# Strided and local attention in blocks of 64 keys instead of tiles of up to 128, ahead of two MoE stages

## The chip, the cores and the metric

The kernel runs as one program on one core of a Trainium2 chip. The metric is the device time of one execution in microseconds (us). The core has TensorE (PE; its weight loads are listed as PEld), VectorE (DVE), ScalarE (ACT) and GpSimd (POOL), which run side by side and are ordered by semaphores alone, and a sync queue (SP) that issues most DMA transfers.

## The reference

Three stages follow each other, all in fp32. The change is in the first.

```python
B, H, S, D = 4, 8, 576, 64
scores = (q @ k.transpose(0, 1, 3, 2)) / sqrt(D)
rel = pos[:, None] - pos[None, :]
mask_local = (rel >= 0) & (rel < 32)                        # heads 0 to 3
mask_strided = (rel >= 0) & (pos[None] % 32 == pos[:, None] % 32)   # heads 4 to 7
attn = softmax(where(mask, scores, -1e9))                   # sum + 1e-9
x = (attn @ v), heads side by side: (2304, 512)
# MoE: 8 experts, top 1, 512 -> 1024 -> 512, tokens with x @ w_skip <= 0 pass through
# then x @ w_in (512 x 2048), a piecewise activation, @ w_out (2048 x 512)
```

A query of a local head sees at most 32 keys. A query of a strided head sees the positions up to its own in its class modulo 32, at most 18. The host lays the strided heads out by class, so that the 18 positions of a class are neighbours and the mask is a block diagonal of 18 by 18 triangles.

## The kernel before, in words

Attention takes a tile of queries against a tile of keys for the four heads of one kind. A local tile is 96 queries against the 128 keys from 32 before them, 6 tiles a batch. A strided tile holds 6 or 5 classes (`CLASSES`), that is 108 or 90 queries against the same 108 or 90 keys, 6 a batch. Two neighbouring tiles are the work of one step (`TWINS`), so a batch has `TB` = 6 steps and the kernel 24.

For each step TensorE does four things. `scores` writes the mask (0 or -8e9) into the score banks by 4 bf16 matmuls against an identity and adds 8 matmuls q·k over 64 partitions; the two halves `hh` of the partitions hold two heads. `turn` transposes the 8 weight blocks, 4 a tile, into `probT_b`. `values` does 8 matmuls of 64 weight columns (the head's dimension) against the transposed weights into `out_b[i % 2]`. Round s of `steps` does `turn(s - 3)`, `scores(s)`, `values(s - 3)` in this order (`LAG` = 3). The first five rounds and the last are written out, the others are a loop with six rounds in its body.

Around it, for step n: VectorE takes the negative row maxima of the 8 blocks (line 604), scales them (606), adds 1e-9 to the sums (611), inverts them (613) and copies the transposed weights to `probT` (620). ScalarE does 8 exponentials with bias and accumulated sum (489) and places the output in `XT` (497); for strided tiles the destination is scattered, one element in 32. GpSimd multiplies the weights by the inverse sums, once a tile (407). The scores of step n wait for the exponentials of step n - 2 (two pairs of banks), `values(n)` for the placing of step n - 2 (two output banks).

The sync queue loads q and k of the local heads, v of the local heads, then the same of the strided heads, each into a single buffer; a buffer of the next batch is requested when the last step that reads it has been scored or multiplied. The routing (logits from line 868 on), the experts (927, 937) and the last stage (970, 983) follow in order on TensorE. The first routing matmul waits for the placing copy of the last step.

The change touches the constants at the top, the buffers of attention, the sync queue's loads, the loops of all five engines over the steps, and the masks of `host_constants`.

## Time and profile before

| what | value |
|---|---|
| time, median of 3 runs | 706.28 us (704.29 to 706.91) |
| the profiled execution, its time | 704.93 us |
| its span, first to last instruction | 703.2 us |
| mean granted clock of TensorE | 0.963 of full speed |
| busy share: TensorE, VectorE, ScalarE, GpSimd | 93%, 47%, 33%, 21% |
| bytes moved by DMA | 73.95 MB |

The span is 1.7 us shorter than the time of the same execution. A busy share is a mean over the whole span; attention is about its first 93 us, and there the shares differ much from the rest. In the profile "x16" counts instructions; an fp32 matmul of the code appears as two of them, a transpose or a bf16 matmul as one. The clock column gives the share of 2.4 GHz that TensorE was granted; 0.5 is 1.2 GHz.

### The profile page before, as it was taken

Reading aid. Unit: us, or ns where it says so; the run is one execution under the profiler, and the core shown is the slowest. Engines: PE = TensorE matmul, PEld = TensorE weight load, DVE = VectorE, ACT = ScalarE, POOL = GpSimd, SP = SyncE. Lnnn points to the kernel's source line nnn. Section 1 sums busy time; section 2 is a strip of 40 time slices with the busy share of each in tenths; the row PEclk is TensorE's granted clock in tenths of the full one; section 3 lists DMA queues with packets and bytes.
Section 4 is the critical chain, followed back from the end, with each engine's and each line's share of the span. In section 5 each row is a group of like instructions: output and inputs, shape, how many; then the busy total and the mean of one; then the engine's idle time right before and its main releaser. Section 6 shows DMA issues by size and latency. Waiting matters only on the chain.

```text
span 703.2 us, 11023 instructions
## 1 busy us (share of the span) xinstructions
PE 657.1 (93%) x4149; PEld 567.4 (81%) x4149; DVE 330.2 (47%) x614; ACT 229.0 (33%) x693; POOL 149.3 (21%) x163
## 2 busy tenths in 40 slices
PE   7999892299999999989999999999999999999995
PEld 4877762299999999968888888888888888888994
DVE  3877733032111112387445644456445564455653
ACT  4999932032111111122223322233222332222331
POOL 1655506302221222785000200002000020000201
PEclk8999977599999999999999999999999999999998
DMA  8565166693777776222000100001000010000100
GB/s 259 180 214 207 40 255 261 225 394 126 265 263 248 262 264 225 88 94 60 1 1 0 61 1 0 1 0 60 0 0 0 0 60 0 0 0 1 61 1 30
DMA packets 37854, 73.95 MB, mean 105 GB/s; under 512 B 2739, under 2 KB 16224, under 8 KB 37808
## 3 DMA queue, kind: packets, MB, share of 16 engines
q1 hardware_dynamic: 34936, 63.92, 26.3%
q0 software_dynamic: 2880, 9.52, 3.5%
q8 instruction: 24, 0.39, 0.2%
q14 instruction: 14, 0.11, 0.1%
HBM read 63.49 MB, written 9.94 MB: 104 GB/s over the span
## 4 chain that ended last, share of the span: by engine, by line
PE 82%; ACT 6%; DMA 4%; POOL 3%; issue 2%; DVE 2%; SPq 0%; DVEq 0%
PE pair L970 28%; PE pair L983 15%; PE bank L983 12%; PE pair L927 10%; PE bank L937 9%; ACT prob L489 5%; DMA WE<-w 2%; POOL x_sorted L418 2%; PE bank L841 1%; PE bank L827 1%; PE bank L911 1%; PE pair L814 1%; PE bank L868 1%; DMA k_loc<-kT 1%; ACT XT L497 1%
## 5 line engine op out<-in xcount | busy, mean ns | idle before, releaser
L970 PE MATMUL pair<-yh,WIH 128*128 128x512 f32 (+1 forms) x320 | 116.5, 371 | 0.2 <-ACT yh L548 0.2
L970 PE MATMUL pair<-yh,WIL 128*128 128x512 f32 (+1 forms) x320 | 116.3, 370 | 0.0
L572 ACT ACTIVATE cl<-cl,half 128x512 f32<-128x512 f32 (+1 forms) x80 | 54.5, 681 | 187.2 <-DVE cl L768 187.2
L477 POOL DMA_INDIRECT out<-XT,tok x18 | 18.8, 1045 | 351.6 <-DVE XT L756 347.7
L776 DVE TENSOR_TENSOR gl<-gr,gh 128x512 fp32r<-128x512 f32 (+1 forms) x80 | 56.3, 703 | 73.1 <-ACT gh L581 71.9
L768 DVE TENSOR_SCALAR cl<-pair 128x512 f32<-128x512 f32 (+1 forms) x80 | 50.9, 637 | 71.0 <-PE pair L970 70.8
L970 PE MATMUL pair<-yl,WIH 128*128 128x512 f32 (+1 forms) x320 | 79.9, 370 | 2.1 <-DVE yl L747 2.1
L927 PE MATMUL pair<-xw,WE 128*128 128x168 f32 x512 | 75.7, 310 | 0.3 <-DMA WE<-w 0.3
L927 PEld LDWEIGHTS pair<-xw,WE 128*128 128x128 f32 x512 | 74.5, 193 | 0.7 <-DMA WE<-w 0.6
L581 ACT CAST gh<-gr 128x512 fp32r<-128x512 f32 (+1 forms) x80 | 46.3, 578 | 85.7 <-PE bank L983 58.3
L937 PE MATMUL bank<-hid,WE 128*128 128x168 f32 x512 | 74.1, 306 | 0.0
L937 PEld LDWEIGHTS bank<-hid,WE 128*128 128x128 f32 x512 | 73.3, 190 | 0.0
L970 PEld LDWEIGHTS pair<-yh,WIH 128*128 128x128 f32 x320 | 60.8, 190 | 11.3 <-ACT yh L548 0.6
L970 PEld LDWEIGHTS pair<-yh,WIL 128*128 128x128 f32 x320 | 60.7, 190 | 10.6
L489 ACT ACTIVATE prob<-pair,sm 96x128 f32<-96x128 f32 (+2 forms) x192 | 65.7, 419 | 10.5 <-DVE sm L606 9.4
L970 PEld LDWEIGHTS pair<-yl,WIH 128*128 128x128 f32 x320 | 57.0, 189 | 13.0 <-DVE yl L747 3.1
L774 DVE TENSOR_TENSOR gr<-gr,cl 128x512 f32<-128x512 f32 (+1 forms) x80 | 52.6, 657 | 22.6 <-ACT cl L572 22.6
L983 PE MATMUL pair<-WOH,gh 128*128 128x512 f32 x160 | 62.5, 391 | 0.0
L983 PE MATMUL pair<-WOL,gh 128*128 128x512 f32 x160 | 62.4, 390 | 0.0
L983 PE MATMUL pair<-WOH,gl 128*128 128x512 f32 x160 | 62.3, 389 | 0.0
L728 DVE TENSOR_TENSOR ytmp<-bank,gb 128x168 f32<-128x168 f32 x32 | 10.6, 333 | 105.6 <-PE bank L937 105.6
L529 ACT ACTIVATE hid<-pair 128x168 f32<-128x168 f32 x64 | 19.9, 310 | 109.7 <-PE pair L927 109.7
(124 smaller groups left out, 933.7 us busy)
## 6 DMA issues: line engine op xcount, KB each, us to landing
WE<-w SPq DMA_DIRECT2D x16, 2048.0 KB, 9.1
xrow<-x_sorted SPq DMA_DIRECT2D x6, 781.5 KB, 10.5
raw_in<-win SPq DMA_DIRECT2D x16, 256.0 KB, 9.2
raw_out<-wout SPq DMA_DIRECT2D x16, 256.0 KB, 2.5
v_loc<-vl SPq DMA_DIRECT2D x4, 768.0 KB, 5.1
q_str<-qT SPq DMA_DIRECT2D x4, 576.0 KB, 5.8
k_str<-kT SPq DMA_DIRECT2D x4, 576.0 KB, 6.8
q_loc<-qT SPq DMA_DIRECT2D x3, 576.0 KB, 4.6
```

Of the source, the lines that this page charges most:

```text
L477: pool.indirect_dma_start(out, bass.IndirectOffsetOnAxis(tok[:, GT * g + t:GT * g + t + 1], 0), rows_of(g, t), None).then_inc(out_done if ...
L489: last = act.activation(prob[0:q, i % 3, e * kk:(e + 1) * kk], score_b[i % 2][0:q, e // 4, e % 4 * kk:(e % 4 + 1) * kk], ACT.Exp, bias=sm[ ...
L529: act.activation(hid[:, par, f, :], hid_b[f % 2][:, 0:WIN], ACT.Relu).then_inc(h_done, 1)
L572: act.activation(cl[:, 0:n], cl[:, 0:n], ACT.Square, bias=half[:, :], scale=0.5).then_inc(squared, 1)
L581: act.copy(gh[:, f % 2, 0:n], gr[:, 0:n]).then_inc(g_high, 1)
L768: dve.tensor_scalar(cl[:, 0:n], h2_b[f % 2][:, 0:n], -1.0, 1.0, ALU.max, ALU.min).then_inc(clamped, 1)
L774: dve.tensor_tensor(gr[:, 0:n], gr[:, 0:n], cl[:, 0:n], ALU.add).then_inc(g_ready, 1)
L776: dve.tensor_tensor(gl[:, f % 2, 0:n], gr[:, 0:n], gh[:, f % 2, 0:n].bitcast(F32), ALU.subtract).then_inc(g_low, 1)
L927: last = pe.matmul(hid_b[f % 2][:, 0:WIN], WE1[:, par, c, P * f:P * (f + 1)], xw[:, buf, c, :], start=(c == 0), stop=(c == DC - 1))
L937: last = pe.matmul(y_b[c][:, 0:WIN], WE2[:, par, f, P * c:P * (c + 1)], hid[:, par, f, :], start=(f == 0), stop=(f == FEC - 1))
L970: last = pe.matmul(h2_b[f % 2][:, 0:tokens], w[:, c, P * f:P * (f + 1)], x[:, c, 0:tokens], start=(k == 0), stop=(k == 3 * DC - 1))
L983: last = pe.matmul(fin_b[t][:, :], x[:, f % 2, P * t:P * (t + 1)], w[:, f, :], start=(f == 0 and k == 0), stop=(f == FFC - 1 and k == 2))
```

## The change

Attention is cut differently. Keys come in blocks of 64 (`KEYS`). Local queries come in blocks of 32 (`BLOCK`), each against the 64 keys that end with them; strided queries in strips of 3 classes, 54 queries (`STRIP`), against 64 keys of which 54 are their own. A step now holds for each of 4 heads two halves `j` of 64 key columns, and in each half the rows of 2 strips, of 4 local blocks, or of a mix (the rest step: one strip, one local block, one single class). So the score tile is always 128 rows by 8 x 64 columns. A batch has 5 steps: two of strips, one rest, two of blocks; the kernel has 20.

- TensorE: 4 mask matmuls of 128 columns a step; 16 score matmuls in a step of strips, 24 in the rest step, 32 in a step of blocks, each of 64 moving columns and 54, 18 or 32 weight columns; 4 transposes of 128 by 128; as many value matmuls as score matmuls, each over 64 partitions with 64 weight columns and 54, 32 or 18 moving columns. The values of step n come in round n + 4, one round after its transposes.
- ScalarE: one exponential over 512 elements from SBUF; the copy of the transposed weights; the placing, in one to three copies.
- VectorE: row maxima of the scores, a subtraction of the maxima from the scores into `prob`, a sum of the exponentials, the add of 1e-9 and the inverse.
- GpSimd: one multiplication a step.
- Score banks: two pairs, used in the order 0, 1, 0, 0, 1 over the five steps; a pair is free once it has been subtracted. The output has one pair of banks instead of two single ones. `prob` has five slots, `probT` three, `probT_b` one bank.
- Loads: strided q and k first, whole inputs per batch in single buffers, v of the local heads (1 MB instead of 0.77) later than before, v of the rest step apart. Constants and the MoE gate's weights are requested during the second batch.
- The loops over steps of ScalarE, VectorE, GpSimd and of the sync queue are written out; TensorE's is a loop with five rounds in its body.

```diff
+BLOCK, KEYS = 32, 64
+BLOCKS = S // BLOCK
+STRIP = 3 * PHASE
+PAIR = 2 * STRIP
...
+SCORES_IN = [0, 1, 0, 0, 1]
+TB = len(TILES_OF)
+STEPS = B * TB
...
-LAG = 3
+SLOTS = TB
+LAG, LAST = 3, 4
...
+            for b in range(1, B):
+                done = TB * (b - 1)
+                sp.wait_ge(scored, done + REST_STEP + 1)
+                load_qk_strided(b)
+                if b > 1:
+                    sp.wait_ge(pv_done, done)
+                    load_v_local(b - 1)
+                sp.wait_ge(scored, done + TB)
+                load_qk_local(b)
+                sp.wait_ge(pv_done, done + STRIPS_B + 1)
                 load_v_strided(b)
+                sp.wait_ge(pv_done, done + REST_STEP + 1)
+                load_v_rest(b)
...
+            for n in range(STEPS):
                 pool.wait_ge(inverted, n + 1)
...
+                pool.tensor_tensor(weights, weights, sm[:, n % SLOTS, 24:32].unsqueeze(2).to_broadcast([P, 8, KEYS]), ALU.mult).then_inc(normed, 1)
...
+            def exps(n):
+                act.wait_ge(lowered, n + 1)
+                act.activation(prob[:, n % SLOTS, :], prob[:, n % SLOTS, :], ACT.Exp, scale=SCALE).then_inc(probs_done, 1)
+
+            def copy_turned(n):
+                act.wait_ge(turned, n + 1)
+                behind(act, pv_done, n - 1)
+                act.copy(probT[:, TURNED_IN[n % TB], :], probT_b[:, :]).then_inc(turn_copied, 1)
...
+            for s in range(STEPS + LAST):
+                if 0 <= s - 1 < STEPS:
+                    exps(s - 1)
+                if 0 <= s - LAG < STEPS:
+                    copy_turned(s - LAG)
+                if 0 <= s - LAST:
+                    place(s - LAST)
...
+                dve.tensor_reduce(small[:, 0:8].rearrange("q (h g) -> q h g", h=2), scores, AX_X, ALU.max).then_inc(maxed, 1)
                 dve.wait_ge(maxed, n + 1)
...
+                dve.tensor_tensor(prob[:, n % SLOTS, :].rearrange("q (h g k) -> q h g k", g=4, h=2), scores,
+                                  small[:, 0:8].rearrange("q (h g) -> q h g", h=2).unsqueeze(3).to_broadcast([P, 2, 4, KEYS]), ALU.subtract).then_inc(lowered, 1)
...
+            def scores_of(i, hh):
+
+                out = score_b[SCORES_IN[i]][:, hh, :]
+                half_ = slice(KEYS * hh, KEYS * hh + KEYS)
+                for j, (mask, _) in enumerate(TILES_OF[i]):
...
+                for j, (_, parts) in enumerate(TILES_OF[i]):
+                    for p in range(2):
+                        for x in parts:
+                            queries, keys = (q_str, k_str) if x.kind == "s" else (q_loc, k_loc)
+                            col = P * p + KEYS * j
+                            yield pe.matmul(out[x.row:x.row + x.queries, col:col + KEYS], queries[half_, p, x.first:x.first + x.queries], keys[half_, p, x.keys:x.keys + KEYS],
+                                            start=False, stop=(j == 1 and p == 1), skip_group_check=True)
...
+                behind(pe, lowered, n if i == BLOCKS_A else n - 1)
+                for _, last in zip(scores_of(i, 0), scores_of(i, 1)):
+                    pass
...
+                for g in range(4):
+                    last = pe.transpose(probT_b[:, P * g:P * (g + 1)], prob[:, i, P * g:P * (g + 1)], ident)
...
+                pe.wait_ge(turn_copied, n + 1)
+                behind(pe, x_placed, n)
...
+                for p in range(2):
                     for hh in range(2):
...
+                        for pair in zip(*(parts for _, parts in TILES_OF[i])):
+                            for j, x in enumerate(pair):
+                                half_, h = slice(KEYS * j, KEYS * (j + 1)), 2 * p + hh
...
+                                last = pe.matmul(out_b[KEYS * hh:KEYS * (hh + 1), j, to:to + x.queries], vv[half_, x.index, HD * h:HD * (h + 1)],
+                                                 probT[half_, TURNED_IN[i], from_:from_ + x.queries], start=True, stop=True)
...
+                if turning:
+                    turn(*turning[:2])
+                if scoring and i != BLOCKS_A:
+                    scores(n, i, b)
+                if valuing:
+                    values(*valuing)
+                if scoring and i == BLOCKS_A:
+                    scores(n, i, b)
```

## Rows read from the trace of the kernel before

**Rows 1.** The page: its busy shares, and one line of its DMA issues.

```profile
PE 657.1 (93%) x4149; PEld 567.4 (81%) x4149; DVE 330.2 (47%) x614; ACT 229.0 (33%) x693; POOL 149.3 (21%) x163
...
k_str<-kT SPq DMA_DIRECT2D x4, 576.0 KB, 6.8
```

**Rows 2.** The chain that ended last: start us, length us, what.

```profile
49.94 1.58 ACT prob L489 x9
...
69.26 1.58 ACT prob L489 x9
...
92.08 0.77 ACT XT L497
...
169.00 9.12 PE bank L937 x64
```

**Rows 3.** Busy time of each engine by stretches of attention.

```profile
core 0: us, PE busy (x) PEld busy (x) DVE busy (x) ACT busy (x) POOL busy (x), PEclk, DMA share, GB/s
...
0.00:9.70 9.70, 6.05 (x30) 2.63 (x30) 2.17 (x6) 1.88 (x4) 1.06 (x8) 0.96 0.75 234
9.40:16.00 6.60, 6.26 (x43) 4.90 (x44) 1.85 (x5) 4.28 (x26) 1.35 (x2) 0.52 1.04 330
16.00:87.00 71.00, 67.44 (x956) 55.75 (x954) 55.94 (x135) 69.87 (x382) 40.95 (x45) 1.00 0.47 161
87.90:98.00 10.10, 8.98 (x68) 4.70 (x68) 1.31 (x4) 1.54 (x2) 0.96 (x2) 0.52 0.45 165
```

**Rows 4.** Timeline of TensorE over one step: start us, length us, instruction.

```profile
29.07 0.60 PE L806 MATMUL pair<-mask_b,ident_b 96*96 96x256 bf16 x4
...
29.60 1.12 PE L814 MATMUL pair<-k_loc,q_loc 64*96 64x128 f32 x16
...
30.65 0.84 PE L841 MATMUL bank<-probT,v_str 90*64 90x90 f32 x16
...
31.42 0.82 PE L827 MATMUL bank<-con,prob 90*90 90x90 f32 x8
...
32.19 0.42 PE L806 MATMUL pair<-mask_b,ident_b 96*96 96x256 bf16 x2
```

**Rows 5.** Timeline of four TensorE groups without their first pair or record.

```profile
39.55 0.73 PE L814 MATMUL pair<-k_str,q_str 64*90 64x90 f32 x14
...
36.31 0.83 PE L814 MATMUL pair<-k_str,q_str 64*108 64x108 f32 x14
...
30.78 0.71 PE L841 MATMUL bank<-probT,v_str 90*64 90x90 f32 x14
...
31.54 0.71 PE L827 MATMUL bank<-con,prob 90*90 90x90 f32 x7
```

**Rows 6.** Timeline: a group's first two weight loads, then its first four.

```profile
36.13 0.17 PEld L814 LDWEIGHTS pair<-k_str,q_str 64*108 64x108 f32 x2
...
36.13 0.27 PEld L814 LDWEIGHTS pair<-k_str,q_str 64*108 64x108 f32 x4
...
40.20 0.14 PEld L841 LDWEIGHTS bank<-probT,v_loc 128*64 128x64 f32 x2
...
40.20 0.20 PEld L841 LDWEIGHTS bank<-probT,v_loc 128*64 128x64 f32 x4
```

**Rows 7.** Groups by line and shape: busy us, mean ns of one, idle before.

```profile
L407 POOL TENSOR_TENSOR prob<-prob,sm 96x512 f32<-96x512 f32 x24 | 24.5, 1039 | 27.8 <-DVE sm L613 27.8
...
L604 DVE TENSOR_REDUCE sm<-pair 96x8 f32<-96x1024 f32 x12 | 14.7, 1221 | 13.1 <-PE pair L814 13.1
...
L868 PE MATMUL bank<-XT,wgs 128*32 128x512 f32 x32 | 5.9, 906 | 0.9 <-ACT XT L497 0.9
...
L497 ACT COPY XT<-bank 128x360 f32 x6 | 5.0, 840 | 0.0
...
L613 DVE RECIPROCAL sm<-sm 96x8 f32<-96x8 f32 x12 | 2.4, 199 | 0.4
...
L572 ACT ACTIVATE cl<-cl,half 128x512 f32<-128x512 f32 x64 | 46.3, 724 | 166.2 <-DVE cl L768 166.2
L774 DVE TENSOR_TENSOR gr<-gr,cl 128x512 f32<-128x512 f32 x64 | 45.7, 715 | 17.2 <-ACT cl L572 17.2
```

More of the change, by code:

```diff
@@ L1 @@
+import itertools
+from collections import namedtuple
 from contextlib import ExitStack
@@ L222, in program @@
         block = ctx.enter_context(nc.Block())
-        STEPS = B * TB
-        FIRST = LAG + 2
-        LOOPS = (STEPS - FIRST) // TB
-        def steps(eng, step, lag):
-            for s in range(FIRST):
-                step(s, s, 0)
-            with eng.Fori(0, LOOPS) as b:
-                for i in range(TB):
-                    step(FIRST + i, TB * b + (FIRST + i), b)
-            for s in range(FIRST + LOOPS * TB, STEPS + lag):
-                step(s, s, 0)
         def rows_of(g, t):
@@ L615, in copy_turned @@
-            def copy_turned(n, i):
-                behind(dve, pv_done, n)
-                for j in range(2):
-                    q, kk, _, _, _, _ = TWINS[i][j]
-                    dve.wait_ge(turned, 2 * n + j + 1)
-                    dve.tensor_copy(probT[0:kk, j, 0:4 * q], probT_b[j][0:kk, 0:4 * q]).then_inc(turn_copied, 1)
-            def step(k, s, b):
-                for lag, work in ((LAG, copy_turned), (0, maxima), (1, inverses)):
-                    m = s - lag
-                    if isinstance(m, int) and not 0 <= m < STEPS:
-                        continue
-                    work(m, (k - lag) % TB)
@@ L629, in _ @@
-            steps(dve, step, LAG)
+                dve.tensor_scalar(small[:, 16:24], small[:, 8:16], 1e-9, None, ALU.add).then_inc(guarded, 1)
+                dve.wait_ge(guarded, n + 1)
+                dve.reciprocal(small[:, 24:32], small[:, 16:24]).then_inc(inverted, 1)
+            for s in range(STEPS + 1):
+                if s < STEPS:
+                    maxima(s)
+                if s >= 1:
+                    inverses(s - 1)
             done = [0]
@@ L818, in turn @@
-            def turn(n, i, b):
-                for j in range(2):
-                    q, kk, _, _, _, _ = TWINS[i][j]
-                    pe.wait_ge(normed, 2 * n + j + 1)
-                    behind(pe, turn_copied, 2 * n + j - 1)
-                    for hh in range(2):
-                        for p in range(2):
-                            e, h = 4 * hh + 2 * j + p, 2 * hh + p
-                            last = pe.transpose(probT_b[j][0:kk, h * q:(h + 1) * q], prob[0:q, i % 3, e * kk:(e + 1) * kk], ident[0:q, 0:q])
-                    last.then_inc(turned, 1)
@@ L845, in step @@
-            def step(k, s, b):
-                for lag, work in ((LAG, turn), (0, scores), (LAG, values)):
-                    m = s - lag
-                    if isinstance(m, int) and not 0 <= m < STEPS:
-                        continue
-                    work(m, (k - lag) % TB, b + (k - lag) // TB)
-            steps(pe, step, LAG)
+            def scores_of(i, hh):
+                out = score_b[SCORES_IN[i]][:, hh, :]
+                half_ = slice(KEYS * hh, KEYS * hh + KEYS)
+                for j, (mask, _) in enumerate(TILES_OF[i]):
+                    pe.matmul(out.rearrange("q (p j k) -> q p j k", p=2, j=2)[:, :, j], ident_b[:, :], mask_b[:, mask, :].unsqueeze(1).to_broadcast([P, 2, KEYS]),
+                              start=(j == 0), stop=False, skip_group_check=True)
+                    yield
+                for j, (_, parts) in enumerate(TILES_OF[i]):
[5 more added lines that the diff above has]
+                                            start=False, stop=(j == 1 and p == 1), skip_group_check=True)
@@ new lines, in round_of, with step @@
+            def round_of(scoring, turning, valuing):
+                n, i, b = scoring
+                if turning:
[6 more added lines that the diff above has]
+                    scores(n, i, b)
+            def step(s):
+                return (s, s % TB, s // TB) if 0 <= s < STEPS else None
+            for s in range(FIRST):
+                round_of(step(s), step(s - LAG), step(s - LAST))
@@ L855, in _ @@
+            with pe.Fori(0, LOOPS) as b:
+                for k in range(FIRST, FIRST + TB):
+                    round_of(*((TB * b + k - lag, (k - lag) % TB, b + (k - lag) // TB) for lag in (0, LAG, LAST)))
+            for s in range(STEPS, STEPS + LAST):
+                if step(s - LAG):
+                    turn(*step(s - LAG)[:2])
+                values(*step(s - LAST))
             pe.wait_ge(wg_in, 16)
```

289 lines of the change are left out of this document (148 added, 141 removed).

## The prediction

> **What bounds the kernel now.** I read the busy shares first [rows 1]: TensorE is busy 93% of the span, but as an average over stages with different limits. The chain of waits [rows 2] then places the change: attention ends with the placing copy at 92.08 + 0.77 = 92.85 us, and the routing matmuls start right behind it. All after that (703.2 − 92.85 = 610.3 us) is untouched and hangs on that copy, so the question is only when attention ends. Between the same point of two batches lie 69.26 − 49.94 = 19.32 us for 6 steps, 3.22 us a step, and the chain stands there on ScalarE's exponentials. The table by stretches [rows 3] shows that two engines share this limit: from 16 to 87 us ScalarE is busy 69.9 and TensorE 67.4 of 71 us, VectorE 55.9, GpSimd 41.0. A gain on ScalarE alone would buy almost nothing: TensorE's own work in a step, from one mask matmul to the next, is 32.19 − 29.07 = 3.12 us [rows 4]. So the sum must be made on TensorE.
>
> **How TensorE's work is priced.** An fp32 matmul of the code leaves two records (8 matmuls are x16 [rows 4]). Alone, a record of 168 columns takes 9.12/64 = 0.1425 us [rows 2], two clock cycles a column at 2.4 GHz. Matmuls on different halves of the array run side by side: scores and values go in pairs of records, and a pair of 90 columns takes (0.71 − 0.24)/6 = 0.078 us [rows 5], the time of one transpose record of 90 columns (last row, 0.078). With 90 weight columns the pair takes (0.73 − 0.24)/6 = 0.082, with 108 (0.83 − 0.26)/6 = 0.095. The weight loads say what limits small ones [rows 6]: the second pair of loads comes 0.10 us behind the first for 108 weight columns, 0.06 for 64. That is about 0.9 ns a column for a pair, twice one load at 2.4 GHz, beside a matmul or not.
>
> **The change, part by part.**
>
> *ScalarE.* Eight exponentials with their accumulator reads, which with one placing copy fill today's step, become one over 512 elements: 0.72 us by the 512-element activation [rows 7]. It takes over from VectorE the copy of the transposed weights (512 elements too, 0.72 at most) and keeps the placing; 360 scattered elements take 0.84 [rows 7], so two copies of 216 about 1.0. Worst step 2.5 us.
>
> *VectorE.* The maximum falls from 1.22 us (1,024 elements) to about 0.69 by its slope of one element per 1.04 ns [rows 7]; added are a subtraction of 512 (0.72), a sum of 512 (0.69), and the small add and the reciprocal remain (0.2 each [rows 7]). With handovers 2.5 us a step. GpSimd's two multiplications of 1.04 [rows 7] become one. None of these three reaches TensorE's new time below, and that is the work that hides them; they bound the step at 2.5 us from below.
>
> *TensorE.* Steps fall from 24 to 20, but a batch has 120 score and 120 value matmuls where it had 48 and 48: 480 records, 96 a step on average (64 in steps of strips, 96 in the rest step, 128 in blocks), against 32. Fixed parts of a step:
> - 4 mask matmuls of 128 columns: half of 0.108, 0.22 us.
> - 4 transposes of 128 columns: 0.078 × 128/90 = 0.11 each, 0.44 (before 0.62).
> - Four changes between groups. Four groups cost 3.12 us, of which 4 × 0.108 + 8 × 0.109 (their columns at 2.4 GHz) + 8 × 0.078 + 8 × 0.078 = 2.55 is pace; 0.57 is change. I take 0.53.
>
> Together 1.19. The value records carry 64 weight columns and only 32 or 54 moving ones, so the load decides: 0.06 a pair, 0.029 a record (they go through two halves at a time). It is bounded below by the moving columns (0.0145 for 32) and above by today's pace, 0.039. The score records carry 32 or 54 weight columns for 64 moving ones. If no more than a pair overlaps, they cost (64 × 2/2.4 + 3)/2 = 0.028; but the code walks them over 4 tiles of the array in strips and 8 in blocks, and four tiles do overlap in this trace: 32 records of 512 columns are done in 5.9 us, mostly at 1.2 GHz, where one alone would take 0.85 [rows 3, 7]. Then loads set 0.013 to 0.025. I take 0.0145, since that row is the nearest to it, and keep 0.028.
>
> P, the step, is 1.19 + 48 × 0.029 + 48 × 0.0145 = 3.28 us. So the step is no shorter than before; the gain comes from having four fewer of them and from ends.
>
> The Trainium skill, page "TensorE: Matmul & The Clock Gate", section "Wait — 56ns, not 53.3ns?", says that matmuls never start closer than some 25 ns however few their columns. The trace shows pairs starting almost together, but none of its averages is under 39 ns, so it doesn't decide. By that figure the step would be 1.19 + 48 × 0.029 + 48 × 0.025 = 3.78 us, close to the pairs-only rival.
>
> *Values one round behind.* Values of step n now follow a round after its transposes, so the copy between them hides behind a whole round of TensorE. That this buys much is excluded by TensorE's idle time, 3.6 us in 71 for all waits together [rows 3]; and it costs nothing while ScalarE has the time. The one output pair makes a loop: values (at most 1.9), last matmul's latency 0.25, placing 0.6 to 1.0, 0.2 of handovers: 2.9 at most, under P with the turn and scores between. The scores of the first block step reuse the rest step's banks and wait for VectorE's 1.45 us; turn and values (1.9) stand ahead of them. Hidden; if that cover went, 1 us a batch.
>
> *Loads.* 4.2 MB a batch instead of 3.6, in 5P = 16.4 us: 258 GB/s. Queries and keys (1.15 MB) have 2.7 rounds, 8.9 us, between their release and need; the later of the two lands 6.8 us after issue in the median [rows 1]. Hidden. The sync queue waits between them for events of earlier rounds alone.
>
> *The ends.* Start: before, the second step began when 1.40 MB of requests had landed, at 9.7 us. Now its data is as much, but the third step needs 2.53 MB: at the 330 GB/s of that stretch [rows 3], 3.4 us later, 13.1. At half clock (0.52 there) its scores end near 15.5, VectorE lowers them 1.5 us later, and the fourth step's scores end near 18.3. From there to the end of the twentieth step's scores are 15.5P. Tail: the last step then needs lowering, exponentials, sums, GpSimd (about 5.0 with handovers), turn 0.7, and behind it two block value groups with their placings (1.9 + 0.8 + 2.2 + 0.7, partly beside), together 11.6.
>
> Sum: 18.3 + 15.5 × 3.28 + 11.6 = 80.7 us against 92.85: 12.1 us less. The profiled execution took 704.93 (span 703.2 and 1.7 around it), which is 1.35 under the median of the three runs shown, 706.28. So 692.8 on its own basis, 694 against that median.
>
> **Rivals.**
> 1. *Pairs only.* Score records overlap no deeper than today. For it: every group of scores and values in the trace runs in pairs. Against: the four-tile routing matmuls. P = 1.19 + 48 × 0.057 = 3.93, end 90.8, total 704.2: no change that can be measured.
> 2. *Deeper overlap.* Loads of different tiles run beside each other and value records cost their columns (0.018), scores 0.0145. P = 2.75, tail about 1.4 shorter: end 71.1, total 684.5.
> 3. *Slower: the pace of a record doesn't fall.* If the stream of instructions, not the columns, sets 0.039 us a record, P = 1.19 + 96 × 0.039 = 4.93 and attention ends at 106.3: 719.8 on the median's basis. It decides from the point where the average record costs 0.030 us: 15.5P = 62.95, P = 4.06. For it: no group of the trace ever went faster on average, and the forecast's value records (0.029) alone stand at that point. Against: in the trace each pace is explained by columns or weights.
> 4. *Loads come late.* The local queries and keys are queued behind 1 MB of values. If they land 2 us late in each of the three later batches, 6 of the 12 us go: 700.
>
> **How the numbers follow.** Forecast (P 3.0 to 3.8, total 690 to 702) 0.50; deeper overlap 0.15; pairs only 0.16; slower 0.12; late loads 0.07. The predicted time is the first's, 694. About half a per cent (3.5 us) is what a measurement of this kernel can tell from no change. Below 702.7 lie the forecast, deeper overlap, most of late loads: 0.72. Within 3.5 us of 706.3 lie pairs only, with edges of others: 0.15. Above: 0.13. The range goes from deeper overlap (684) to just above pairs only (708), and leaves out the slow rival and the far side of the second, about 0.17.
>
> **What would show each step.** In the new profile attention should end near 81 us, and a batch take 16.4. The score records of a block step should need some 0.9 to 1.1 us for 64, the values 1.9 for 64; strips 0.5 to 0.8 and 0.95 for 32. If scores take 1.8, rival 1; if both take 2.5, rival 3. ScalarE should be busy about 2.1 and VectorE 2.5 us a step, neither on the chain in steady steps. The third step's scores should wait for the local keys until about 13 us, and TensorE for no later load. What makes me wrong is above all the price of a small record, since 480 of them a batch multiply any error: 1 ns in it is 1.5 us of the total.

## The result and the profile after

The changed kernel takes 699.8 us (median of 20 runs, 695.58 to 704.51), the kernel before beside it 704.29 (20 runs): ratio 0.9931, 95% interval 0.9912 to 0.9951. It is faster, and clear of noise: 0.69% of the time before is 4.9 us, and the two medians differ by 4.5. The forecast was 12 us. A second series, e0_again below, gives 0.9929. The profile comes from one execution of 701.6 us, 1.8 above the median.

The page of the changed kernel, its span and its busy shares, and behind it one table by stretches: the start, the first batches, the start of TensorE's loop, one steady batch.

```profile
span 699.8 us, 12450 instructions
PE 642.5 (92%) x5173; PEld 557.1 (80%) x5173; DVE 316.7 (45%) x570; ACT 188.8 (27%) x361; POOL 126.1 (18%) x135
```

```profile
core 0: us, PE busy (x) PEld busy (x) DVE busy (x) ACT busy (x) POOL busy (x), PEclk, DMA share, GB/s
9.40:16.00 6.60, 4.86 (x88) 3.26 (x88) 2.35 (x5) 0.64 (x2) 1.04 (x1) 0.55 1.05 358
16.00:36.00 20.00, 17.65 (x532) 14.35 (x524) 14.09 (x30) 9.51 (x20) 6.25 (x6) 0.81 0.61 193
36.00:46.00 10.00, 6.01 (x180) 4.99 (x177) 4.20 (x8) 2.46 (x6) 1.04 (x1) 0.74 0.65 229
52.30:69.10 16.80, 14.33 (x524) 12.17 (x522) 11.52 (x26) 9.10 (x20) 5.21 (x5) 1.00 0.89 274
```

In the steady batch (52.3 to 69.1 us) no engine is full: ScalarE, 98% busy before [rows 3], is busy 54%, TensorE 85%, where it had been 95%. From 36 to 46 us TensorE is busy only 60%, and the granted clock is 0.74 of full speed in the mean; it is at half from 40.8 to 47.6 us.

The chain of waits, first through one steady round and then at the end of attention (start us, us, what):

```profile
58.21 1.17 PE pair L840 x58
59.37 0.02 issue
59.40 0.70 DVE sm L643
60.10 0.02 issue
60.12 0.69 DVE prob L646
60.81 0.60 DVE sm L652
61.41 0.02 issue
61.44 0.18 DVE sm L654
61.62 0.02 issue
61.64 0.21 DVE sm L656
61.86 0.07 issue
61.92 1.05 POOL prob L440
62.98 0.12 issue
63.10 0.65 PE bank L860 x4
...
89.30 0.59 ACT XT L539
89.89 0.14 issue
90.03 4.50 PE out_pair L925 x48
```

Attention ends at 89.89 us, 2.96 earlier than the 92.85 of [rows 2]; what follows takes 609.9 us (610.3 before). And the chain no longer stands on ScalarE but runs through VectorE and GpSimd: the sum (L652) and the inverse of one step stand on VectorE behind the maxima and the subtraction (L643, L646) of the next.

TensorE's timeline (start us, length, instruction, in brackets the idle time before it): a score group in the loop's first pass, then in the steady batch the rest step's scores in part, value and score groups of block steps, the turn at which that chain ends, and a strip step.

```profile
36.34 0.82 PE L840 MATMUL pair<-k_loc,q_loc 64*32 64x64 f32 x61
41.08 0.42 PE L840 MATMUL pair<-k_loc,q_loc 64*32 64x64 f32 x3 [3.91 <-issue]
...
52.30 0.32 PE L840 MATMUL pair<-k_str,q_str 64*54 64x64 f32 x4
52.55 0.25 PE L840 MATMUL pair<-k_loc,q_loc 64*32 64x64 f32 x2
...
53.03 0.25 PE L840 MATMUL pair<-k_loc,q_loc 64*32 64x64 f32 x2
...
53.52 0.25 PE L840 MATMUL pair<-k_loc,q_loc 64*32 64x64 f32 x2
...
54.24 1.46 PE L882 MATMUL out_pair<-probT,v_loc 64*64 64x32 f32 x64
...
60.10 0.86 PE L840 MATMUL pair<-k_loc,q_loc 64*32 64x64 f32 x64
60.89 0.72 PE L882 MATMUL out_pair<-probT,v_str 64*64 64x54 f32 x32
63.10 0.65 PE L860 MATMUL bank<-con,prob 128*128 128x128 f32 x4 [1.49 <-POOL prob L440]
63.59 0.39 PE L832 MATMUL pair<-mask_b,ident_b 128*128 128x128 bf16 x4
63.91 0.67 PE L840 MATMUL pair<-k_str,q_str 64*54 64x64 f32 x32
```

About 0.2 us of each length is the last matmul's latency. So 64 score records of this block step start within 0.64 us, 10 ns apart (in the batch's other block step, at 58.14 us, within 1.00 us, 16 ns apart), and 64 value records within 1.24 us, 20 ns apart. The records of block and strip steps are cheaper than forecast. The first two rows show the surprise: TensorE stops for 3.91 us between two records of one group, with no semaphore to wait for ("issue").

### The profile page after: what moved, and what is told of

It is laid out like the page before. It is cut to its first block, busy times and chain, and to the rows that moved or that the text cites. A ratio compares the mean times of both kernels' runs of the same rounds, so it can differ in the third digit from the quotient of the medians.

```text
span 699.8 us, 12450 instructions
## 1 busy us (share of the span) xinstructions
PE 642.5 (92%) x5173; PEld 557.1 (80%) x5173; DVE 316.7 (45%) x570; ACT 188.8 (27%) x361; POOL 126.1 (18%) x135
## 4 chain that ended last, share of the span: by engine, by line
PE 87%; DVE 4%; POOL 3%; DMA 2%; issue 2%; ACT 1%; SPq 1%; DVEq 0%
PE pair L1027 28%; PE pair L1040 16%; PE bank L1040 12%; PE pair L984 11%; PE out_pair L994 5%; PE bank L994 5%; PE pair L840 2%; PE out_pair L882 2%; POOL x_sorted L449 2%; PE bank L860 2%; DMA k_loc<-kT 1%; POOL prob L440 1%; DVE sm L643 1%; DVE prob L646 1%; PE out_pair L925 1%
## 5 line engine op out<-in xcount | busy, mean ns | idle before, releaser
L809 DVE TENSOR_TENSOR gl<-gr,gh 128x512 fp32r<-128x512 f32 (+1 forms) x80 | 54.6, 682 | 73.3 <-ACT gh L622 72.2
L804 DVE TENSOR_SCALAR gr<-pair 128x512 f32<-128x512 f32 (+1 forms) x80 | 50.2, 627 | 0.0
L1040 PE MATMUL bank<-WOH,gh 128*128 128x512 f32 x128 | 49.8, 389 | 0.0
L1040 PE MATMUL bank<-WOL,gh 128*128 128x512 f32 x128 | 49.8, 389 | 0.0
L1040 PE MATMUL bank<-WOH,gl 128*128 128x512 f32 x128 | 49.8, 389 | 0.0
```

What stands on the lines that cost most here:

```text
L804: dve.tensor_scalar(gr[:, 0:n], h2_b[f % 2][:, 0:n], 1.0, -1.0, ALU.max, ALU.add).then_inc(over, 1)
L809: dve.tensor_tensor(gl[:, f % 2, 0:n], gr[:, 0:n], gh[:, f % 2, 0:n].bitcast(F32), ALU.subtract).then_inc(g_low, 1)
L1040: last = pe.matmul(fin_b[t][:, :], x[:, f % 2, P * t:P * (t + 1)], w[:, f, :], start=(f == 0 and k == 0), stop=(f == FFC - 1 and k == 2))
```

## The experiments

They take up what the trace shows: TensorE's half clock (1.2 instead of 2.4 GHz) from 10.1 to 23.7 us and behind the stall (40.8 to 47.6 us), the stall itself, VectorE's order, the rest step, and the values one round behind. All kernels are the changed kernel with the edit shown. "Ratio" is against the kernel before in the same series, with its 95% interval; one interval is 2 to 3 us to either side, and the difference between an edit and the changed kernel carries about 3 us either way. The kernel before had medians of 704.1 to 705.7 us in these four series, so gains by medians and by ratios differ by about 1 us at most. By times alone e3, e4, e7, e10, e14 and e15 differ from the changed kernel; e2 and e8 hardly do, and e1, e5, e6, e9 and e11 not clearly. The last column but one is the distance between the first rest-step score matmuls of neighbouring batches (in the changed kernel 13.13, 30.13, 52.30 and 69.08 us), then from the last of these to the end of attention.

| run | median us | ratio | batch distances, us | attention ends |
|---|---|---|---|---|
| changed kernel | 699.80 | 0.9931 | 17.00, 22.17, 16.78, 20.81 | 89.89 |
| e0_again | 699.58 | 0.9929 (0.9896 to 0.9961) | 17.88, 20.59, 16.87, 20.25 | 88.68 |
| e1_late_v | 700.33 | 0.9923 (0.9894 to 0.9952) | 16.71, 20.93, 17.19, 20.65 | 88.68 |
| e2_inverse_first | 696.81 | 0.9890 (0.9859 to 0.9920) | 17.00, 22.16, 16.30, 18.93 | 87.30 |
| e3_rest_grouped | 694.50 | 0.9847 (0.9816 to 0.9878) | 16.12, 17.84, 16.35, 21.99 | 85.00 |
| e4_same_round | 705.50 | 1.0011 (0.9984 to 1.0038) | 20.47, 19.55, 17.56, 22.10 | 93.07 |
| e5_busy_fill | 696.50 | 0.9900 (0.9868 to 0.9932) | 15.41, 20.03, 16.69, 19.65 | 84.87 |
| e6_values_order | 697.46 | 0.9896 (0.9856 to 0.9937) | 16.54, 20.94, 16.23, 20.67 | 87.11 |
| e7_unrolled | 704.97 | 1.0000 (0.9978 to 1.0021) | 17.53, 21.58, 21.05, 24.83 | 97.86 |
| e8_all | 696.43 | 0.9874 (0.9836 to 0.9912) | 14.66, 23.49, 17.53, 20.32 | 89.33 |
| e9_all_but_dve | 697.28 | 0.9890 (0.9852 to 0.9929) | 14.80, 20.71, 16.21, 20.14 | 85.87 |
| e10_tail_fill | 692.66 | 0.9828 (0.9797 to 0.9858) | 14.79, 23.20, 16.80, 16.87 | 84.32 |
| e11_scores_two_tiles | 695.24 | 0.9886 (0.9849 to 0.9924) | 15.76, 18.00, 17.14, 19.69 | 82.95 |
| e12_small_loads | | | 16.70, 18.14, 16.42, 20.46 | 85.69 |
| e13_all_small_loads | | | 13.59, 17.26, 13.99, 16.87 | 74.48 |
| e14_all_late_v | 689.93 | 0.9793 (0.9769 to 0.9817) | 16.89, 19.43, 15.75, 16.86 | 81.86 |
| e15_late_v_old_dve | 691.06 | 0.9811 (0.9785 to 0.9838) | 15.91, 19.64, 16.08, 17.59 | 82.03 |

The distances are of one profiled execution each and scatter: the second holds the stall, which differs from one execution to the next (3.91 us in the first row; 0.49 in e0_again, with another of 1.26 us before its second rest step), while the third, the steady batch, agrees in the first two rows within 0.1 us.

**e0_again**: no edit.

> The changed kernel once more, unchanged. In its first profile TensorE stood still for 3.9 us in the middle of a group of score matmuls (37.2 to 41.1 us), with no semaphore to wait for, and fell to half clock behind it. Theory A (the instruction stream ran dry, because a 16 KB packet of instructions landed late): the stall recurs at the same place of the program, its length may differ, and with it attention's end (89.9 us). Rival (an accident of one execution): no stall, attention ends some 4 to 6 us earlier. Ratio to the kernel before as measured, 0.993.

The same time and the same steady batch. The stall recurs at its place in the program, but there with 0.49 us only.

**e1_late_v**: the sync queue requests the 1 MB of local values behind the local queries and keys.

```diff
+                sp.wait_ge(scored, done + TB)
+                load_qk_local(b)
                 if b > 1:
                     sp.wait_ge(pv_done, done)
                     load_v_local(b - 1)
-                sp.wait_ge(scored, done + TB)
-                load_qk_local(b)
```

> The sync queue requests the local values of the batch before (1 MB) after the next local queries and keys instead of ahead of them, so that nothing large is requested around 36 us. Theory A with this cause (the instruction packet queues behind that 1 MB, 2.9 us at 350 GB/s): the stall of 3.9 us goes or shrinks below 1 us, the half clock behind it too, attention ends 4 to 6 us earlier, ratio to before near 0.986. Rival (the stall belongs to the first pass through the loop whatever is in flight): it stays at 3 to 4 us, ratio 0.993.

No change, and the stall stays (3.92 us, until 40.82). It doesn't hang on that one transfer.

**e2_inverse_first**: in the first block step's round VectorE sums and inverts the step before ahead of the maxima.

```diff
+                first = s % TB == BLOCKS_A and s < STEPS
+                if first:
+                    inverses(s - 1)
                 if s < STEPS:
                     maxima(s)
-                if s >= 1:
+                if s >= 1 and not first:
                     inverses(s - 1)
```

> On VectorE, in the round of the first block step, the sums and inverses of the step before come ahead of the maxima, and not behind them. Theory B (the turn of the rest step waits 1.5 us a batch, because its inverses are queued behind maxima that wait for scores issued last in their round): this wait of 1.5 us goes, a steady batch falls from 16.8 to 15.3 us, total 3 to 5 us less, ratio near 0.987. Rival (the chain is only shifted, and the next turn waits the longer): a batch stays at 16.8, ratio 0.993.

The wait of the turn falls from 1.49 to 0.39 us, the steady batch only by 0.5 and not by 1.5 as expected. The rest reappears: in this batch the masks' weight loads wait 0.5 us for the later subtraction, and the masks twice for keys that are still loading (0.4 and 0.2 us). The 2.8 us in the medians are hardly clear of noise.

**e3_rest_grouped**: the rest step's scores are issued by width, first all of 54 columns, then those of 32 and 18.

```diff
-                for j, (_, parts) in enumerate(TILES_OF[i]):
+                for own in ((slice(0, 1), slice(1, 3)) if i == REST_STEP else (slice(0, 4),)):
+                  for j, (_, parts) in enumerate(TILES_OF[i]):
...
-                        for x in parts:
+                        for x in parts[own]:
```

> In the rest step the score matmuls of 54 weight columns come first and those of 32 and 18 after them, instead of changing between them 8 times. Theory C (each change of the tile's width costs about 0.15 us; the group takes 1.79 us for 48 records against 0.64 for 64 in a block step): the group falls to 0.7 to 0.9 us. In the total up to 4 us less if TensorE is what a batch waits for there, and nothing if VectorE's chain takes the time up. Rival (small matmuls of 18 columns are slow themselves): the group stays above 1.5 us.

In the changed kernel the group runs from 52.30 to the values at 54.24, 1.94 us, its records in four clusters 0.5 us apart (52.55, 53.03, 53.52 and 54.00 us). With the edit it has one change of width, and the values follow 1.16 us behind its start (timeline of TensorE, e3_rest_grouped; between the rows single records of alternating tiles):

```profile
46.66 0.66 PE L841 MATMUL pair<-k_str,q_str 64*54 64x64 f32 x16
47.25 0.25 PE L841 MATMUL pair<-k_loc,q_loc 64*32 64x64 f32 x2
47.26 0.23 PE L841 MATMUL pair<-k_str,q_str 64*18 64x64 f32 x2
...
47.82 1.40 PE L883 MATMUL out_pair<-probT,v_loc 64*64 64x32 f32 x62
```

0.78 us a batch, 3.1 in four, of the 5.1 us gained. The remaining 2 lie within the interval; the stall was also short here (1.45 us, no half clock behind it). The other theory, that records of 18 columns are slow themselves, is out: the same records are now done in 1.16 us. The Trainium skill, page "TensorEngine Tiling (Array Packing)", section "Key Properties", says that the engine drains when the way of tiling changes. The trace agrees with such a cost: seven changes of width (54 against 32 and 18 columns) take 0.78 us more than one, 0.13 for each of the six.

**e4_same_round**: values in the round of their own transposes.

```diff
-LAG, LAST = 3, 4
+LAG, LAST = 3, 3
```

> The value matmuls of a step are issued in the same round as its transposes, not one behind. My theory: the copy of the transposed weights (0.72 us, 1.1 with latency and handovers) lies open where only a round's masks and scores (1.1 us) or, in the round of the first block step, nothing stands between the turn and the values; some 1.1 us a batch and a few tenths in other rounds, 5 to 7 us over four batches, less one round of 1.5 us in the tail: 3 to 5 us slower than the changed kernel, about 703.5. Rival: the turns wait for VectorE's and GpSimd's chain anyway (2.4 us of waits a batch), so the new wait only takes the place of those and the tail is a round shorter: 0 to 2 us faster, 698 to 700.

5.9 us slower by the medians, 5.6 by the ratios: the whole gain is gone, and more was lost than the 3 to 5 us expected. In one steady batch TensorE now waits for the copy (waits from 53.4 to 71 us, total, times, longest), and hardly any more for GpSimd:

```profile
PE out_pair L882 <- ACT probT L521: 2.3, 2, 1.1
...
PE bank L860 <- POOL prob L440: 0.3, 1, 0.3
```

The batch is 0.8 us longer. Between the first two rest steps, in part at half clock, it is 3.5 us longer; there 1.8 us are a stall like the one above (until 31.66 us) and no wait for the copy.

**e5_busy_fill**: idle matmuls keep TensorE busy through the waits of the start.

```diff
             for s in range(FIRST):
                 round_of(step(s), step(s - LAG), step(s - LAST))
+                for _ in range((10, 7, 7, 0, 0)[s]):
+                    pe.matmul(bank[3][:, :], warm[:, 0:P], warm[:, :], start=True, stop=True)
```

> 10, 7 and 7 idle matmuls of 512 columns (into a bank that nothing reads) follow the first three rounds, where TensorE waits for loads and for the first lowered scores. My theory: the half clock from 10 to 24 us costs about 3 us, because the rounds between 16 and 24 us run at it; with the engine kept busy through the waits the clock stays at full and the last values end 2 to 3 us earlier: about 697. Rival: those rounds wait for VectorE, GpSimd and ScalarE and not for TensorE's own pace, so the clock there costs nothing: 699 to 700.5, with the granted clock up all the same.

By the medians 3.1 us, as forecast, but 2.1 by the ratios, so the times alone don't prove it; the trace does show it at work. The first batch distance is 15.41 us, against 17.0 and 17.9 in the changed kernel's two traces and 16.7 in e1, whose edit doesn't touch the first batch. From 16 to 25 us first the changed kernel, then this one (same columns as above):

```profile
16.00:25.00 9.00, 8.06 (x230) 6.46 (x226) 7.01 (x15) 3.51 (x8) 2.08 (x2) 0.57 0.61 212
```

```profile
16.00:25.00 9.00, 7.32 (x264) 6.04 (x263) 7.64 (x17) 5.25 (x11) 3.13 (x3) 1.00 0.77 300
```

Full clock (2.4 GHz) instead of mostly half, and more matmuls done in less busy time (264, 4 of them idle ones, against 230). In the changed kernel the clock had fallen at 10.1 us, amid the waits for the first loads (the local keys until 12.55).

**e6_values_order**: the value matmuls walk over all four quarters of the array.

```diff
                 for p in range(2):
-                    for hh in range(2):
-                        for pair in zip(*(parts for _, parts in TILES_OF[i])):
+                    for pair in zip(*(parts for _, parts in TILES_OF[i])):
+                        for hh in range(2):
```

> The value matmuls walk over all four quarters of the array in turn instead of staying on two of them for four matmuls. My theory: a quarter needs 58 ns for a record of 64 weight columns, so 64 records on four quarters can be done in 16 x 0.058 = 0.93 us, and the old order gets only 1.24 because now and then two quarters stand idle; 0.3 us off each block step, 0.1 off strips, 0.8 a batch, 3 us in all: about 696.5. Rival: the order makes no difference, since the engine already starts each record when its quarter is free (64 in 1.24 either way): 699 to 700.5.

```profile
52.15 1.13 PE L882 MATMUL out_pair<-probT,v_loc 64*64 64x32 f32 x64
53.21 0.66 PE L860 MATMUL bank<-con,prob 128*128 128x128 f32 x4
```

The next group starts 1.06 us behind the first value instead of 1.38 (54.24 to 55.62 in the changed kernel), so 0.32 us less: as expected from one record per 58 ns and quarter. In the time the 2.3 us (ratios) are not clear of noise.

**e7_unrolled**: TensorE's loop is written out.

```diff
-            with pe.Fori(0, LOOPS) as b:
-                for k in range(FIRST, FIRST + TB):
-                    round_of(*((TB * b + k - lag, (k - lag) % TB, b + (k - lag) // TB) for lag in (0, LAG, LAST)))
+            for s in range(FIRST, STEPS):
+                round_of(step(s), step(s - LAG), step(s - LAST))
```

> TensorE's loop over the later batches is written out, so every batch's instructions are new ones. My theory: the stall of 1 to 4.7 us in the loop's first pass comes from instructions that arrive just in time (the 16 KB instruction packets), and passes two and three have none because they run from what is already there; written out, each batch gets such stalls, 1 to 4 us each, and instruction packets go on past 45 us: 2 to 7 us slower, 702 to 707. Rival: the stall belongs to entering the loop; written out there is none at all: 3 us faster, about 696.5.

Slower by 5.0 us (ratios; 5.4 by the medians). The traced execution, 710.42 us, is one of its longer ones, and has half clock also from 53.1 to 63.3 us. Stalls now come in every batch, two of them here:

```profile
81.30 0.43 PE L840 MATMUL pair<-k_loc,q_loc 64*32 64x64 f32 x26 [1.54 <-issue]
...
85.23 0.32 PE L882 MATMUL out_pair<-probT,v_str 64*64 64x54 f32 x3 [1.31 <-issue]
```

The DMA queues of the instructions tell the rest (packets, MB, share), from 46 to 80 us first in this kernel, then in the changed one:

```profile
q8 instruction: 7, 0.11, 1.3%
q14 instruction: 2, 0.02, 0.1%
```

```profile
q14 instruction: 2, 0.02, 0.1%
```

Queue q8 moved 7 packets of 16 KB here and none in the changed kernel. The loop's second and third pass run from what has been fetched; the first pass doesn't. So the stall is a wait for instructions. It also fits in time. In all the traces together TensorE stands still 41 times between 20 and 90 us for over 0.4 us with no semaphore to wait for, never in the kernel before. In 38 cases it goes on 1.2 to 1.6 us after a packet of q8 has landed (in the changed kernel landed at 39.77 us, on at 41.08; in e8_all 33.89 and 35.21, 42.34 and 43.78). Three short ones, two of 0.5 us in e4 and one of 0.7 in e14, have no such packet and stay unexplained.

**e8_all, e9_all_but_dve, e10_tail_fill**: e2, e3, e5 and e6 together; the same without e2; and the four with idle matmuls in the last rounds as well.

```diff
                 values(*step(s - LAST))
+                for _ in range((4, 3, 3, 0)[s - STEPS]):
+                    pe.matmul(bank[3][:, :], warm[:, 0:P], warm[:, :], start=True, stop=True)
```

> Four edits together: inverses ahead of the maxima in the first block step's round, the rest step's scores grouped by width, the idle matmuls of the first three rounds, and the value matmuls over all four quarters. Alone they gave 2.8, 5.1, 3.1 and 2.1 us. My theory: they act on different places (VectorE's chain, two groups of TensorE, the clock of the start), so most of it adds up, but a batch that gets shorter on TensorE waits more for VectorE and GpSimd: 8 to 11 us faster than the changed kernel, 689 to 692. Rival: all of them fill the same slack, VectorE's and GpSimd's chain and the instruction stream set the pace, and no more than the best of them is seen: 693.5 to 695.

> The same without the edit to VectorE's order. My theory: with the shorter groups on TensorE the wait of the turn behind the first block step (1.5 us) stays or grows, so this is 3 to 4 us slower than with it: 692 to 695.5. Rival: that wait moves elsewhere as it did in part when the edit stood alone, and the two are within 1.5 us.

> All four edits, and 4, 3 and 3 idle matmuls of 512 columns in the waits of the last rounds. My theory: the half clock that begins in the last rounds (from 82 or 79 us) costs the last values (2.3 against 1.1 us for 64) and the first routing matmuls 1 to 2 us; with the waits filled it doesn't come: 1 to 2 us under the kernel with the four edits. Rival: the clock is already full there in the faster kernel, as in the run with the fill at the start alone, and the idle matmuls gain nothing: within 1 us.

The edits don't add up: 3.2 us together by the medians (4.0 by the ratios) where 13.1 would be their sum, worse than my theory, and no more than e3 alone gave. Two things took it. The stalls grew (in e8_all 1.79 and 5.93 us, until 35.21 and 43.78): a faster TensorE only reaches the missing instructions sooner. And the loads became late (timeline of e10_tail_fill, at the masks of a strip step):

```profile
61.06 0.60 PE L835 MATMUL pair<-mask_b,ident_b 128*128 128x128 bf16 x4 [1.46 <-DMA k_str<-kT]
```

With and without VectorE's new order no difference can be measured. The filled tail is worth 3.8 us by the medians, at the edge of the intervals and more than expected. From the last masks to the end of attention e10 takes 11.2 us, and so does e8 (11.0), in whose profiled execution the clock was full there anyway; where it was at half for most of it, e9 and e6 took 14.4 and 14.2, and the changed kernel, with half clock from 81.7 to 85.2 us alone, 13.7. So the half clock in the tail costs up to 3 us when it comes. With the fill the full clock held until 17 us or more past the end of attention in all four traces (e10, e13, e14, e15); without it half clock came before that end in nine of thirteen.

**e11_scores_two_tiles**: the scores of one tile of the array one behind the other.

```diff
-                for j, (_, parts) in enumerate(TILES_OF[i]):
-                    for p in range(2):
-                        for x in parts:
+                for group in zip(*(parts for _, parts in TILES_OF[i])):
+                    for j, x in enumerate(group):
+                        for p in range(2):
```

> The score matmuls of one tile of the array stand one behind the other (8 records) before the next tile's, so that only two tiles work at a time; nothing else changes. My theory: a tile takes one record per 56 ns whatever runs beside it, the 10 ns of a block step's record come from eight tiles at once, and with two the 64 records take 1.8 us instead of 0.64, the 32 of a strip step 0.9 instead of 0.45: 3 to 3.5 us a batch, less the 2.4 us of waits that this partly fills: 5 to 12 us slower than the changed kernel, 705 to 712, so that the change would gain nothing. Rival: the engine looks far enough ahead to start the other tiles anyway, or the price is the instruction stream's and not the tiles': within 2 us of 699.6.

```profile
51.43 1.42 PE L840 MATMUL pair<-k_loc,q_loc 64*32 64x64 f32 x64
52.78 0.66 PE L860 MATMUL bank<-con,prob 128*128 128x128 f32 x4
```

A miss against both theories. The group is slower, 64 records in some 1.2 us, 19 ns each, so the order does set the price, but not the 28 ns of two tiles alone: the engine starts some of the next tile's records. The steady batch is 0.4 us longer. Yet the kernel was faster by 3 to 4 us, which the intervals just fail to separate from nothing. In its trace the half clock lasted from 8.3 to 15.1 us instead of 10.1 to 23.7, and the only stall in the loop's first pass was 0.9 us. That the longer groups kept TensorE busier there and that this is the reason is argued; no run isolates it.

**e12_small_loads, e13_all_small_loads**: the loads of queries, keys and values of batches 1 to 3 are cut to a small part, in the changed kernel and in e10_tail_fill. These batches compute with stale data, and everything behind attention takes longer (727.4 and 715.0 us in all), presumably because tokens go to other experts; only attention can be read.

```diff
-                sp.dma_start(q_loc[:, :, :], qT[b, 0]).then_inc(qk_loc_in, 16)
+                n = KEYS if b else S
+                sp.dma_start(q_loc[:, :, 0:n], qT[b, 0, :, :, 0:n]).then_inc(qk_loc_in, 16)
...
-                sp.dma_start(v_loc[:, :, :], vl[b, :, 0:LOC]).then_inc(v_loc_in, 16)
+                n = 1 if b else LOC
+                sp.dma_start(v_loc[:, 0:n, :], vl[b, :, 0:n]).then_inc(v_loc_in, 16)
```

> The changed kernel, with the loads of queries, keys and values of batches 1 to 3 cut to a small part (64 of their columns, one of the value blocks), so that these batches compute with stale data; all instructions and waits stay. Theory A: the instruction packet in the loop's first pass lands late because 2 to 3 MB of loads are under way from 34 to 44 us (300 to 400 GB/s); with the loads gone the stall falls from 0.8 to 4.7 us to under 0.5 and the time to 695 to 696.5. Theory B, the rival: the fetch itself is too slow for block steps, which use an instruction packet of 16 KB in 2.3 us; the stall stays at 2 to 4 us and the time at 698 to 700.

> The same cut of the loads in the kernel with four edits and the filled tail (692.7). Theory A: its stalls (7.7 us in all) and its wait for late keys (1.5 us) go, a batch takes under 16 us: 683 to 686. Theory B: only the wait for keys goes, the stalls stay: 690.5 to 692.

Both theories hold in part, by one execution each. In e12 one stall of 1.2 us is left, which lies within what the changed kernel shows (0.5 to 3.9). In the faster kernel the difference is plain: e13 has one of 2.0 us, e10 four of 1.4, 1.0, 1.8 and 4.2 from 25 to 43 us, 8.4 in all.

```profile
33.39 0.44 PE L849 MATMUL pair<-k_loc,q_loc 64*32 64x64 f32 x27 [1.97 <-issue]
```

So in the faster kernel most of the stall is an instruction packet that lands late while loads fill the DMA engines (from 36 us on, some 400 GB/s in the changed kernel), and a part is the fetch itself. And without loads e13's steady batch takes 14.0 us at full clock (stretch table):

```profile
43.62:57.61 13.99, 12.29 (x523) 10.72 (x521) 11.90 (x25) 8.67 (x19) 5.22 (x5) 1.00 0.37 96
```

VectorE is at 85%, TensorE at 88%. The changed kernel without loads (e12) takes 16.4 us for the same batch, so once nothing arrives late the four edits are worth 2.4 us a batch; with the loads they gave nothing (17.5 in e8 and 16.8 in e10, against 16.8).

**e14_all_late_v, e15_late_v_old_dve**: e10_tail_fill and its twin without e2, both with e1's order of loads.

> The kernel with four edits and the filled tail, with the 1 MB of local values requested behind the local queries and keys. If late queries and keys are what keeps the four edits from adding up, they land 2 us earlier, the waits of 0.9 to 1.7 us at the masks go, and it is 1 to 3 us faster: 690 to 691.5. Rival: the values then land late instead, or VectorE sets the batch: within 1 us of 692.7.

> The same without the edit to VectorE's order. The batches with it take 16.8 us in the combination, those without it 16.2, so if it is worth nothing there (its wait moves to the masks, which stand behind the same subtraction), this is 0 to 2 us faster than with it: 689 to 691.5. Rival: the edit's gain is real and hidden by a difference between executions: 1 to 2 us slower.

```profile
49.25:65.00 15.75, 12.71 (x523) 10.83 (x521) 11.96 (x26) 8.95 (x20) 5.21 (x5) 1.00 0.85 273
```

The batch falls from 16.80 (e10) to 15.75 us, and the wait for keys in it from 1.5 to 0.7. The edit that was worth nothing alone (e1) seems worth some 2.5 us here: the traces show where, but it is one execution each, and the ratios' intervals overlap a little. e14 is the best version run: 689.93 us, 14.8 less than the kernel before, three times the gain of the change. e2's edit stays undecided beside it.

## Why the prediction was right and wrong

The direction was right and the size wrong, 12 us forecast and 4.9 measured. The step that failed is the stretch of 15.5 steps at one steady price: the forecast put at nothing both the instructions that arrive late in code run for the first time and the half clock that lasts past the start and comes back behind the stall. In the profiled execution attention ended 9.2 us later than the forecast's 80.7: the start 1.2, the step's price 1.2, the stall 3.9, the half clock some 2.0, the tail 0.9. By its own steps:

- *P = 3.28 us a step*: right in sum, 3.36 measured (16.78/5), and wrong in its parts, so the agreement is luck. Score records of blocks cost 10 and 16 ns instead of 14.5, value records 20 instead of 29; strips 14 and 15. Against that the rest step's scores cost 37 ns each, through changes of width that the forecast didn't price. TensorE's work is 14.3 us a batch, 2.9 a step: nearer to rival 2 (2.75) than to the forecast.
- *"None of these three reaches TensorE's new time"*: this failed. VectorE's durations were right (0.70, 0.69, 0.60, 0.18, 0.21 on the chain; five steps 11.5 us a batch) and ScalarE's load was under its 2.1 us a step (1.8). But a share is not a latency. The forecast added up VectorE's work and didn't lay its order beside TensorE's uneven rounds. In the shortest round, sum and inverse stand behind the next step's maxima and subtraction, and the chain shown above ends 1.49 us after TensorE's last work. All waits, 2.5 us a batch, fill what the cheap records freed. But taking that wait away (e2) shortened the batch by 0.5 us only, so this order alone didn't cost the forecast its gain.
- *"That this buys much is excluded by TensorE's idle time"*: this failed too. Values one round behind are worth 5.6 to 5.9 us (e4), the whole gain. The argument used the idle time of the kernel before, where rounds were long enough to hide the copy. What must be asked is what covers a wait in the new rounds: 1.1 us of masks and scores, and in the first block step's round nothing.
- *"From there to the end of the twentieth step's scores are 15.5P"*: the step that failed in size. The stretch took 57.9 us (19.46 to 77.38), not 50.8. At the measured P it would be 52.0; 3.9 us are the stall, and the 2.0 left go to the half clock behind the start and behind the stall (an estimate, by difference). e5, with 2.1 to 3.1 us for the clock in the start, is in line with it; e7, e10 and e13 show that the stall is late instructions. The kernel before has no stall, with 3 instruction packets on q8 up to 40 us where this one has 5. The forecast counted 480 records a batch instead of 192 and never asked whether their instructions arrive in time.
- *Start, 18.3 us*: 19.5. Local keys at 12.55 us (forecast 13.1) were right. *Tail, 11.6*: 12.5, partly at half clock.
- *Rival 1, pairs only*: refuted, 10 and 14 ns a record, up to eight tiles at once. *Rival 3, the instruction stream sets 0.039 us a record*: refuted as a pace, but its mechanism exists as stalls in code that runs for the first time. *Rival 4, loads late*: not in this kernel, whose trace shows no wait for a load behind the start, but as soon as it is made faster (waits for keys of 2.6 us in e8, 1.5 in e10, 0.6 in e2).
- The Trainium skill, page "TensorE: Matmul & The Clock Gate", section "Wait — 56ns, not 53.3ns?", has matmuls never start closer than some 25 ns. This case's trace disagrees for matmuls of different tiles: 64 records start within 0.64 us. Records that return to the same tile follow 56 to 58 ns apart (64 value records on four quarters in e6: 16 rounds in 0.92 us).

What stays open: how much of a stall is fetch and how much contention in a given execution (it varied from 0.5 us in e0_again to 4.5 in e2, both until 41.4 us), and why e11 met so little of it.

## What to carry to other kernels

- Price a change of shape in latency as well as in work: write down for each round what stands in front of each waiting group on every engine. The shortest round decides, not the mean.
- Many small matmuls on different tiles are cheap (10 to 20 ns), if their order walks over the tiles and keeps one width together. Their instructions are not free: in code that runs once, ask whether they arrive, and what loads are under way then.
- Freed time goes to the next limit in line, here VectorE's order, then the instruction stream, then the loads. Edits worth 13.1 us one by one (by medians, three of the four at the edge of the noise or within it) gave 3.2 together; with the tail kept busy and the loads in another order it was 9.7.

## Not expected of the hardware

- TensorE stopped for 0.4 to 5.9 us without any semaphore in code that ran for the first time, and went on 1.2 to 1.6 us after a 16 KB instruction packet had landed (38 waits in 17 traces). Written out, the loop brought 7 such packets from 46 to 80 us and stalls in every batch.
- Score matmuls of eight tiles (64 partitions by 32 columns) started 10 ns apart; a change of tile width cost 0.13 us.
- Idle matmuls in waits that would come anyway gained 2 to 3 us at the start and some 3 in the last rounds, both at the edge of what the times resolve, where the clock stayed at 2.4 GHz instead of 1.2.
